# MLP products in blocks of seven for two token chunks, the third chunk accumulated through PSUM

## What is computed

```python
x = _moe_ref(x=x, **moe_kwargs)
h = x @ w_in              # 1536x512 @ 512x2048
g = h * np.cos(h)
return (g @ w_out)        # 1536x2048 @ 2048x512
```

## Time and profile before

| | |
|---|---|
| median of 3 runs | 792.18 us (790.63 to 792.59) |
| profiled execution | 790.99 us, its span 789.2 us |
| granted TensorE clock | 1.00 over the whole span |
| TensorE matmul busy | 778.2 us, 99% |
| VectorE busy | 665.7 us, 84% |
| ScalarE, GpSimd busy | 365.1 and 363.1 us, 46% each |

### The profile page before, as it was taken

How to read it: one execution, slowest core, us unless ns; L and a number is a source line. 1 busy time by engine, 2 the same in 40 slices (tenths; PEclk the granted TensorE clock), 3 DMA queues, 4 the chain that set the end, 5 groups by cost and what they waited for, 6 DMA issues and landing times.

```text
span 789.2 us, 11824 instructions
## 1 busy us (share of the span) xinstructions
PE 778.2 (99%) x4277; PEld 656.2 (83%) x4277; DVE 665.7 (84%) x1050; ACT 365.1 (46%) x692; POOL 363.1 (46%) x337
## 2 busy tenths in 40 slices
...
DMA packets 20446, 44.86 MB, mean 57 GB/s; under 512 B 2408, under 2 KB 2456, under 8 KB 20388
## 3 DMA queue, kind: packets, MB, share of 16 engines
...
## 4 chain that ended last, share of the span: by engine, by line
PE 93%; DVE 3%; DMA 2%; ACT 1%; issue 1%; SPq 0%; POOL 0%; DVEq 0%; ACTq 0%
PE ps L1294 29%; PE ps L1315 19%; PE ps L1450 17%; PE ps L1431 15%; PE ps L1332 11%; DMA att<-att_in 2%; PE ps L1216 1%; PE ps L1260 1%; PE ps L1230 0%; PE ps L1247 0%; DVE w_sum L1075 0%; DVE w_lo L912 0%; DVE temps L1003 0%; DVE w2s_lo L917 0%; DVE att L871 0%
## 5 line engine op out<-in xcount | busy, mean ns | idle before, releaser
L1294 PE MATMUL ps<-x_hi,w_hi 128*128 128x512 f32 (+1 forms) x448 | 150.6, 336 | 2.3 <-DVE temps L1033 1.0
L1294 PE MATMUL ps<-x_hi,w_lo 128*128 128x512 f32 (+1 forms) x448 | 150.6, 336 | 0.0
L1294 PE MATMUL ps<-x_lo,w_hi 128*128 128x512 f32 (+1 forms) x448 | 150.5, 336 | 0.0
L970 DVE TENSOR_TENSOR y<-ps,y 128x512 f32<-128x512 f32 x216 | 143.0, 685 | 0.0
L569 POOL TENSOR_TENSOR h_lo<-temps,h_hi 128x512 fp32r<-128x512 f32 x64 | 97.9, 1529 | 47.3 <-ACT h_hi L747 47.3
L563 POOL TENSOR_TENSOR h_lo<-temps,h_hi 128x512 fp32r<-128x512 f32 x48 | 70.8, 1475 | 60.3 <-ACT h_hi L741 60.2
L1294 PEld LDWEIGHTS ps<-x_hi,w_hi 128*128 128x128 f32 x448 | 84.7, 189 | 16.0 <-DVE temps L1033 1.6
L1294 PEld LDWEIGHTS ps<-x_lo,w_hi 128*128 128x128 f32 x448 | 84.7, 189 | 11.7
L1294 PEld LDWEIGHTS ps<-x_hi,w_lo 128*128 128x128 f32 x448 | 84.7, 189 | 8.8
L1003 DVE SCALAR_TENSOR_TENSOR temps<-ps,temps 128x512 f32<-128x512 f32 (+1 forms) x96 | 53.0, 552 | 38.8 <-PE ps L1294 38.8
L1450 PE MATMUL ps<-h_hi,w_hi 128*128 128x512 f32 x192 | 74.9, 390 | 0.4 <-DVE w_lo L917 0.4
...
## 6 DMA issues: line engine op xcount, KB each, us to landing
w_raw<-w_in SPq DMA_DIRECT2D x96, 256.0 KB, 2.7
...
out<-y SPq DMA_DIRECT2D x12, 256.0 KB, 2.0
...
temps<-p_scr SPq DMA_DIRECT2D x4, 256.0 KB, 3.7
...
lam<-lam_in SPq DMA_DIRECT2D x1, 6.0 KB, 1.6
```

Source lines behind the costliest of these rows:

```text
L970: dve.tensor_tensor(at, bank, at, ALU.add).then_inc(s_ym, 1)
L1294: mm = pe.matmul(ps[:, bank, 0:CTS[side]], ww[q % 2][:, of], xx[side][:, 2 * x + k, :], start=(opens and k == 0 and n == 0), stop=(k == 1 ...
```

## The change

Everything up to the last expert quarter stays, but for its third chunk, whose last unit now adds in the bank: ScalarE puts y into the bank first, and chunk 2 of x is taken from the bank.

From quarter 18 on the four gates of chunks 0 and 1 (C11, C12, C22, C21) come from seven products of blocks (six matmuls each), with sums of x blocks made once (`x_sum`), sums of weight blocks made each quarter by GpSimd (`v1_sum`), a copy of the first product and two kept products (ScalarE), and two sums on VectorE. Quarters 16 and 17, and the third chunk's gates G0 and G1 in all quarters, stay direct (12 matmuls each). The gates use three banks. The second products of chunks 0 and 1 in quarters 16 to 22 run as chains M1 to M7 in banks 3 to 6, on gates and on four gate sums a quarter (`gate_sum`), with weight sums by GpSimd (`v2_sum`). The third chunk's sums are carried: ScalarE copies y into the bank (`carry_in`), TensorE adds, ScalarE copies back (`carry_out`). The last quarter's second products are 12 direct units. Low halves are divided between VectorE and GpSimd; `high` is ScalarE's. In the diff below (cut to its core and set in to the left) the blocks are: TensorE's products, its order, VectorE's order in the transition and in the quarters, GpSimd's order, ScalarE's order.

```diff
-CHUNK_ORDER = (1, 0, 2)
-GATES = 2 * CHUNKS * MLP_QUARTERS
-LAG = 5
-GATE_BANKS = 4
-GATE_BANK = (1, 2, 0, 3)
-T_RING = 3
+SEVENS = 18
+LAST = ALL_QUARTERS - 1
...
+UP_ORDER = (P1, P5, P2, P6, P3, P7, P4)
+CHAIN_1, CHAIN_2 = (M1, M5, M6, M7), (M3, M2, M4)
...
+def up_product(q, i):
+    w, x, bank, opens = PRODUCTS[i]
+    if i == P1:
+        pe.wait_ge(s_gate, gate_count(q - 1, C21))
+        pe.wait_ge(s_vlo[W1_0], q - QUARTERS)
+        pe.wait_ge(s_vlo[W1_1], q - QUARTERS)
+    elif i == P5:
+        pe.wait_ge(s_gate, gate_count(q - 1, G0))
+        pe.wait_ge(s_vlo[W1_2], q - SEVENS + 1)
+        if q == SEVENS:
+            for n in range(4):
+                pe.wait_ge(s_xtlo[n], 1)
+    elif i in (P2, P6):
+        pe.wait_ge(s_copy, STEPS + q - SEVENS + 1)
+    elif i == P3:
+        pe.wait_ge(s_p5, STEPS + q - SEVENS + 1)
+    elif i == P7:
+        pe.wait_ge(s_u2, STEPS + q - SEVENS + 1)
+    else:
+        pe.wait_ge(s_c22, STEPS + q - SEVENS + 1)
+    for k in range(2):
+        of = slice(FF2 * w + P * k, FF2 * w + P * (k + 1))
+        x_high, x_low = x_block(x, k)
+        for n, (ww, xx) in enumerate(((w1_hi, x_high), (w1_hi, x_low), (w1_lo, x_high))):
+            mm = pe.matmul(ps[:, bank, :], ww[q % 2][:, of], xx, start=(opens and k == 0 and n == 0),
+                           stop=(k == 1 and n == 2), skip_group_check=True)
+    mm.then_inc(s_prod, 1)
...
+def chain_unit(q, j, t):
+    pe.wait_ge(s_glo[j], q - QUARTERS + 1)
+    if j in (M5, M3, M6, M7):
+        pe.wait_ge(s_vlo[W2_2], q - QUARTERS + 1)
+    elif q == QUARTERS:
         pe.wait_ge(s_wlo, wlo_count(q, W2_1))
+    else:
+        pe.wait_ge(s_vlo[W2_0 if j == M1 else W2_1], q - QUARTERS)
+    if j == M1 and q == QUARTERS:
+        pe.wait_ge(s_x2lo2, LOW_LAST[1 + t] + 1)
+    elif j == M1:
+        pe.wait_ge(s_yu2[1 + t], q - QUARTERS)
+    elif j in (M5, M6, M7):
+        pe.wait_ge(s_yq[(M1, M5, M6)[(M5, M6, M7).index(j)]], 2 * (q - QUARTERS) + t + 1)
...
+    hi, lo = m_weights(q, j, t)
+    n = b_slot(q, j)
+    for m, (ww, hh) in enumerate(((hi, h_hi), (hi, h_lo), (lo, h_hi))):
+        mm = pe.matmul(ps[:, M_BANK[j] + t, :], ww, hh[:, n, :], start=(M_OPENS[j] and m == 0),
+                       stop=(m == 2), skip_group_check=True)
+    mm.then_inc(s_chain[j not in CHAIN_1], 1)
...
+def third_chunk(q, d):
     if d == 0:
-        pe.wait_ge(s_glo, 2 * j + 2)
-    if i >= KT:
-        pe.wait_ge(s_y2, i - KT + 1)
+        pe.wait_ge(s_glo[B_G0], q - QUARTERS + 1)
+        pe.wait_ge(s_glo[B_G1], q - QUARTERS + 1)
+    if q > QUARTERS:
+        pe.wait_ge(s_uin, KT * (q - QUARTERS) + d + 1)
+    elif d == 0:
+        pe.wait_ge(s_x2lo2, KT)
+    elif d == 3:
+        pe.wait_ge(s_yu2[0], 1)
+    else:
+        pe.wait_ge(s_yq[M7], d)
     at = slice(P * d, P * (d + 1))
     for f in range(2):
-        for n, (ww, hh) in enumerate(((w2_hi, h2_hi), (w2_hi, h2_lo), (w2_lo, h2_hi))):
-            mm = pe.matmul(ps[:, GATE_BANKS + i % KT, :], ww[:, q % 2, f, at], hh[:, j % CHUNKS, f, :],
+        for n, (ww, hh) in enumerate(((w2_hi, h_hi), (w2_hi, h_lo), (w2_lo, h_hi))):
+            mm = pe.matmul(ps[:, U_BANK[d], :], ww[:, q % 2, f, at], hh[:, split_slot(q, B_G0 + f), :],
+                           start=(q == QUARTERS and f == 0 and n == 0), stop=(f == 1 and n == 2),
+                           skip_group_check=True)
+    mm.then_inc(s_dn, 1)
...
+q = QUARTERS
+m_unit(q - 1, M2, 0)
+m_unit(q - 1, M2, 1)
+u_last(0)
+m_unit(q - 1, M4, 0)
+m_unit(q - 1, M4, 1)
+u_last(2)
+up_direct(q, C12, 0)
+up_direct(q, C12, 1)
+u_last(1)
+up_direct(q, C22, 0)
+up_direct(q, C22, 1)
+up_direct(q, C21, 0)
+up_direct(q, C11, 0)
+up_direct(q, C11, 1)
+u_last(3)
+up_direct(q, C21, 1)
+up_direct(q, G0, 0)
+up_direct(q, G0, 1)
+up_direct(q, G1, 0)
+chain_unit(q, M1, 0)
+chain_unit(q, M1, 1)
+up_direct(q, G1, 1)
+chain_unit(q, M5, 0)
+chain_unit(q, M5, 1)
+for q in range(QUARTERS + 1, ALL_QUARTERS):
+    more = q < LAST
+    first_part(q, 0)
+    chain_unit(q - 1, M3, 0)
+    chain_unit(q - 1, M3, 1)
+    first_part(q, 1)
+    chain_unit(q - 1, M2, 0)
+    chain_unit(q - 1, M6, 0)
+    first_part(q, 2)
+    chain_unit(q - 1, M6, 1)
+    chain_unit(q - 1, M7, 0)
+    first_part(q, 3)
+    chain_unit(q - 1, M7, 1)
+    first_part(q, 4)
+    chain_unit(q - 1, M2, 1)
+    first_part(q, 5)
+    third_chunk(q - 1, 0)
+    third_chunk(q - 1, 1)
+    chain_unit(q - 1, M4, 0)
+    chain_unit(q - 1, M4, 1)
+    first_part(q, 6)
+    third_chunk(q - 1, 2)
+    up_direct(q, G0, 0)
+    up_direct(q, G0, 1)
+    up_direct(q, G1, 0)
+    if more:
+        chain_unit(q, M1, 0)
+    up_direct(q, G1, 1)
+    if more:
+        chain_unit(q, M1, 1)
+        chain_unit(q, M5, 0)
+    third_chunk(q - 1, 3)
+    if more:
+        chain_unit(q, M5, 1)
+for i in range(CHUNKS * KT):
+    last_unit(i)
...
+q = QUARTERS
+w2_piece(q, 0)
+m_add(q - 1, M2, 0)
+m_add(q - 1, M2, 1)
+x2_low(1, 0)
+m_add(q - 1, M4, 0)
+x2_low(1, 1)
+m_add(q - 1, M4, 1)
 combine()
+x2_low_from_bank(0)
+combine_on()
+x2_low(0, 0)
+reduce_first(q, C12)
+x_sum(T1)
+reduce_second(q, C12)
+x2_low(0, 1)
+reduce_first(q, C22)
+x_sum(T3)
+w2_piece(q, 1)
+gate(q, C12)
+reduce_second(q, C22)
+x2_low_from_bank(2)
+x2_low_from_bank(1)
+x_sum(T4)
+reduce_first(q, C11)
+reduce_second(q, C11)
+v2_low(q, 2)
+gate(q, C22)
+x2_low_from_bank(3)
+reduce_first(q, C21)
+gate(q, C11)
+reduce_second(q, C21)
+low(q, M1)
+gate_sum(q, T1)
+x_sum_low(T1)
+gate_sum(q, T2)
+reduce_first(q, G0)
+gate(q, C21)
+reduce_second(q, G0)
+gate_sum(q, T4)
+v1_low(q + 1, 1)
+v1_low(q + 1, 0)
+gate_sum(q, T3)
+low(q, M3)
+x_sum_low(T3)
+reduce_first(q, G1)
+gate(q, G0)
+reduce_second(q, G1)
+low(q, M6)
+x_sum_low(T2)
+y_add(q, M6, 0)
+y_add(q, M2, 0)
+gate(q, G1)
+low(q, M4)
...
+for q in range(QUARTERS + 1, ALL_QUARTERS):
+    sevens, more = q >= SEVENS, q < LAST
+    reduce_first(q, C11)
+    y_add(q - 1, M6, 1)
+    y_add(q - 1, M7, 0)
+    low(q - 1, B_G1)
+    reduce_second(q, C11)
+    low(q - 1, B_G0)
+    if sevens:
+        sum_up_second(q)
+    y_add(q - 1, M7, 1)
+    gate(q, C11)
+    reduce_first(q, C12)
+    if more:
+        a21_low(q + 1)
+    if sevens:
+        sum_up_third(q)
+    reduce_second(q, C12)
+    y_add(q - 1, M2, 1)
+    v2_low(q, 0)
+    reduce_first(q, C22)
+    if more:
+        v1_low(q + 1, 1)
+    reduce_second(q, C22)
+    v2_low(q, 1)
+    gate(q, C12)
+    reduce_first(q, C21)
+    gate(q, C22)
+    if more:
+        gate_sum(q, T1)
+    reduce_second(q, C21)
+    if more:
+        gate_sum(q, T2)
+    y_add(q - 1, M4, 0)
+    reduce_first(q, G0)
+    if more:
+        gate_sum(q, T3)
+    reduce_second(q, G0)
+    if more:
+        y_add(q, M1, 0)
+    y_add(q - 1, M4, 1)
+    if not more:
+        combine_last()
+        combine_last_on()
+    gate(q, C21)
+    if more:
+        y_add(q, M1, 1)
+    reduce_first(q, G1)
+    gate(q, G0)
+    reduce_second(q, G1)
+    if not more:
+        finish(0)
+    low(q, M2)
+    if not more:
+        finish(1)
+    if more:
+        gate_sum(q, T4)
+        y_add(q, M5, 0)
+        y_add(q, M3, 0)
+    gate(q, G1)
+    if not more:
+        finish(2)
+        finish(3)
+    if more:
+        y_add(q, M5, 1)
+        y_add(q, M3, 1)
+    if q + 1 < LAST:
+        v1_low(q + 2, 0)
+    if more:
+        y_add(q, M6, 0)
+        y_add(q, M2, 0)
+low(LAST, B_G1)
+low(LAST, B_G0)
+for i in range(KT, CHUNKS * KT):
+    finish(i)
...
+for q in range(QUARTERS + 1, ALL_QUARTERS):
+    more = q < LAST
+    low(q, M1)
+    if more:
+        v1_sum(q + 1, SUM_3)
+    low(q, M5)
+    low(q, M3)
+    if more:
+        v1_low(q + 1, 2)
+        low(q, M6)
+        low(q, M7)
+    if q + 1 < LAST:
+        v2_sum(q + 1, SUM_1)
+        v2_sum(q + 1, SUM_2)
+        v2_sum(q + 1, SUM_3)
+    if more:
+        low(q, M4)
+    if q + 1 < LAST:
+        v2_sum(q + 1, SUM_4)
+        v2_low(q + 1, 2)
+        v1_sum(q + 2, SUM_1)
+        v1_sum(q + 2, SUM_2)
+        v1_sum(q + 2, SUM_4)
...
+for q in range(QUARTERS + 1, ALL_QUARTERS):
+    sevens, more = q >= SEVENS, q < LAST
+    if sevens:
+        copy_up(q)
+    high(q - 1, M4)
+    v2_high(q, 1)
+    if sevens:
+        keep_up_fifth(q)
+    carry_in(q - 1, 0)
+    turns(q, C11)
+    high(q - 1, B_G1)
+    v2_high(q, 0)
+    if sevens:
+        keep_up_sixth(q)
+    if more:
+        v1_high(q + 1, 1)
+        v2_high(q, 2)
+    sine(q, C11)
+    square(q, C11)
+    turns(q, C12)
+    if more:
+        a21_high(q + 1)
+    carry_in(q - 1, 1)
+    carry_out(q - 1, 0)
+    turns(q, C22)
+    sine(q, C12)
+    carry_in(q - 1, 2)
+    square(q, C12)
+    high(q, M1)
+    sine(q, C22)
+    turns(q, C21)
+    square(q, C22)
+    carry_out(q - 1, 2)
+    carry_out(q - 1, 1)
+    if more:
+        v1_high(q + 1, 2)
+    high(q, M5)
+    turns(q, G0)
+    sine(q, C21)
+    square(q, C21)
+    high(q, M3)
+    carry_in(q - 1, 3)
+    sine(q, G0)
+    turns(q, G1)
+    square(q, G0)
+    if more:
+        high(q, M7)
+    if q + 1 < LAST:
```

(50 more changed lines are left out.)

766 lines of the change are left out of this document (568 added, 198 removed).

## The result

The changed kernel takes **783.68 us** (median of 4 runs, 782.42 to 785.29) against 792.27 (790.63 to 792.59) for the kernel before in the same comparison: ratio 0.9897, 95% interval 0.9873 to 0.9921. It is 8.6 us or 1% faster, and a little less than half of the 17.7 us of matmuls that it leaves out came through. The profiled execution is the slowest of its four (785.29 us, span 783.5). In the experiments' own comparisons the kernel before had medians of 790.7 to 791.5, so a difference of 1 or 2 us between the medians of two variants says little; where it matters, a length counted inside the traces stands beside it.

What follows compares the result with a forecast made beforehand. TensorE was taken to bound the kernel, one matmul after another in the MLP. From the profiled 790.99 us: minus 17.7 for matmuls removed, plus 5.6 for the transition, plus 6.0 for steady quarters, gives 784.9, forecast 785 us; range 774 to 798.

Steps and rivals of the forecast that it cites:

- What is removed, 78 x 0.2267 = 17.7 us: MLP on TensorE: 36 up and 42 down matmuls fewer, each worth its pitch of 0.2267 us, 17.7 us saved.
- VectorE's 27.1 us of work a quarter by the pitch: Steady MLP quarters: VectorE's 44 operations of 512 elements and 2 of 256 take 27.1 of 29.9 us before any wait.
- GpSimd's 17.9: Steady MLP quarters: GpSimd's low halves and weight sums take 17.9 us of 29.9.
- I take the measured 0.17: Steady quarters: meetings with GpSimd cost each of 18 two-SBUF VectorE operations 0.17 us, as in the expert stage; 3.1 a quarter.
- the signs given: Steady quarters, if the forecast holds: about 31 us long, VectorE over 95% busy, gate sums well over 0.68 us.
- Rival 1: Steady quarters: TensorE stays the bound at 29.9 us each, only a smaller transition loss is left; 776 us, chance 0.30.
- The transition, +5.6: From the last expert block to quarter 17's first gate: TensorE loses 4.6 us waiting, some 1.0 for collisions.
- behind C21's start VectorE has fifteen operations ... Idle 2.9: Transition, before G0: VectorE finishes chunk 2's low halves at 540.3, TensorE is there at 537.5; idle 2.9 us.
- The predicted 1.0 for meetings: Transition: GpSimd's x sums of 1024 beside VectorE's operations cost some 1.0 us in collisions.
- Rival 2: Steady quarters: collisions with GpSimd make VectorE the bound, 35.5 us a quarter, 807 us in all; chance 0.18.
- Rival 3: Steady quarters: with three gate banks one late gate delays the next, 3 us a quarter over TensorE's; 794 us, chance 0.10.
- The weight DMAs, costed at nothing: MLP: the same 32 DMAs of 2.7 us on an almost empty queue, with 7 us to spare, cost nothing.

Runs made afterwards that it cites:

- experiment 6: Changed kernel with all up gates direct, seven products in no quarter, 36 matmuls more: 792.46 us, ratio 1.0018.
- experiment 2: Changed kernel with ScalarE's sine and square of C12 moved ahead of turns(C22) and v2_high(q,2) in the transition: 785.32 us, ratio 0.9924.
- experiments 7 and 8: Changed kernel, quarters 18 to 22: VectorE's first reductions done twice (two, then all six), 791.15 and 828.13 us; GpSimd low halves twice (one, then three), 797.52 and 807.25.
- experiments 1 to 4: Changed kernel with the transition's operations reordered on VectorE, ScalarE, both plus two more moves, then all three engines (two versions): 784.01, 785.32, 783.90, 785.45 and 784.80 us.

## Why the prediction was right, and which steps were not

The forecast was 785 us in a range of 774 to 798; measured 783.68. The direction was right, the account of TensorE's gain too. That the number came so close is partly luck: two of its terms were wrong, one 6.0 too high and one 4.4 too low, and they nearly cancel: with 0 for the steady quarters and 10.0 for the transition its sum is 790.99 - 17.7 + 10.0 = 783.3, and 785.3, the profiled execution's own time, with the 2.0 us of the late start.

- **What is removed, 78 x 0.2267 = 17.7 us.** Right, in the count (4199 against 4277) and in the price (experiment 6: 8.0 us inside the traces for 36 matmuls, 0.22 each).
- **VectorE's 27.1 us of work a quarter by the pitch.** Right: 27.7 busy (not the "over 95%" given as a sign, but 93%). GpSimd's 17.9 were 20.1, since the row showed the undisturbed durations and GpSimd does wait here: its low halves take 1.37 in the mean instead of 1.30, and some of its sums of 256 elements 1.12 instead of 0.75.
- **"I take the measured 0.17" for each of 18 two-SBUF operations, and 0.9 us of idle: +6.0 us.** Wrong; it was 0. The meetings were priced as chance at the rate of the expert stage, but the order of the MLP isn't chance: GpSimd's long operations lie beside VectorE's PSUM reads, and where the short ones meet VectorE it is GpSimd that waits. Laying out the new order for GpSimd, as was done for VectorE, might have shown this beforehand. Of the signs given, quarters of about 31 us and gate sums well over 0.68 us did not come (29.92 and 0.686). Rival 1 had the steady part right (29.9 us a quarter, no wait in it), and the forecast's mechanism fails there; rival 1's own 776 fails by the transition.
- **The transition, +5.6.** Too small: 10.0 given back. C21's idle was predicted as 1.5 and was 1.1. The step that failed is G0's: "behind C21's start VectorE has fifteen operations ... Idle 2.9". It was 4.3, from a C21 that itself started 2.2 us later than laid out (532.9, not 530.7). VectorE needed 11.4 us from C21's start to G0's, not 9.6, and the difference is the 1.8 us for which it waited for the sine and square of C12: ScalarE was costed by its sum (it has room), and not by what stands ahead of that sine in its queue. (Taking it away alone brought nothing, experiment 2: it sits in a chain.) Added to this come 1.6 us of low clock, which no row of before hinted at, small waits of 0.5 to 0.7 for ScalarE's copies, h_lo and issue, and the restarts. The predicted 1.0 for meetings was 2.7 on VectorE (0.6, 0.6 and 1.5), of which the 1.5 lie behind G0's start. The whole lies at the upper bound of 10 given there, but not for its reason, that each 1024-wide pair meets.
- **Rival 2**, meetings that make VectorE the bound, 807 us. Its mechanism is real and its price of the right size: experiments 7 and 8 call it up with 1.25 to 4 us of work a quarter and end at 791 to 828 (34.2 us a quarter in the last of them, 35.5 in the rival). What kept it away is where the operations lie against each other, and which of two that meet starts first.
- **Rival 3**, an order that waits for itself. Not in the steady part. In the transition it is what experiments 1 to 4 met: whichever wait was taken away, the next one took its time.
- **The weight DMAs, costed at nothing.** Right: 2.7 us each, and no wait of TensorE for them.

No version that does the whole work is faster than the changed kernel. The two that leave out part of it have lower medians, by 0.9 and 1.6 us, but their ratios of 0.9898 and 0.9887 lie within the interval of its own (0.9897 [0.9873, 0.9921]); inside the traces their stage is 1.3 and 2.0 us shorter. What stays open is whether less work on VectorE in the transition, with nothing left out, would bring back part of the 10 us: GpSimd idles there from 525.3 to 534.7 us, but its operations would meet VectorE's, and giving it the x sums T1 and T3 wasn't tried.
